# Turning x in the DMA, as two planes of 16-bit halves, in a pooled-attention and two-layer expert kernel

## The chip, the cores and the metric

The kernel runs on one core of one Trainium2 chip. A core has five engines that run side by side and wait for one another by semaphores: TensorE (matrix products, PE in the profile), VectorE (DVE), ScalarE (ACT), GpSimd (POOL) and SyncE (SP, which issues DMAs). The metric is the time of one execution in microseconds (us), as the median of several runs. Less is better.

## The reference, cut to what matters

```
s = scale * (q @ k.T);  a = softmax(s);  x = a @ v         # k = v = pooled kv @ w_sr, q is 24576 x 128

# expert layer 1, D = 128, E = 8 experts, F = 1024
logits = x @ w_gate;  e = argmax(logits);  gate = softmax(logits)[e]
x = gate * relu(x @ w1[e]) @ w2[e]

# expert layer 2: the same with its own weights, and one factor more
x = gate * sigmoid(x @ w_output_gate)[e] * relu(x @ w1[e]) @ w2[e]
```

Each token (a row of x, 128 numbers) goes to one expert, the one with the highest logit, and each layer is a pair of products with that expert's weights.

## The kernel before

**Stages.** Attention computes x in 96 blocks of 256 tokens. The two expert layers follow, each as up to 104 tiles of 256 tokens that all belong to one expert; 100 are in use here. Tokens get from the order of the input to the order of the experts through HBM: each row is scattered to a place in its expert's part of a bucket (x_bucket for layer 1, y_bucket for layer 2), and a tile is 256 consecutive rows of a bucket, read back. A row in a bucket is 768 bytes: 128 numbers of x, the token's number (ID) and its gate (GATE), and unused space. The last layer scatters its rows straight to the output.

**Precision by halves.** TensorE multiplies in a rounded 32-bit format. So each operand is kept as a rounded part and a rest (x_hi and x_lo, h_hi and h_lo, the weights likewise), and each product is made of three. ScalarE makes the rounded part (x_high, line 1503; h_high, line 1509), VectorE the rest (x_low, line 1712; h_low, line 1718).

**One tile, on TensorE** (tile_body). The products need x with the 128 features on the partitions, while a bucket's rows come with tokens on the partitions. So turn_x (lines 1279 to 1287) turns the tile's two blocks of 128x128 by two transposes into PSUM bank 5, from which x_high and x_low read. The up products of a tile come in four parts of six matmuls (up, line 1303), the down products in four of six (down, line 1320), then the result, copied by ScalarE to oT (yT_out, line 1517), is turned back into rows (tile_rows, lines 1335 and 1337: in layer 1 by a product that also gives the next layer's logits, in layer 2 by a transpose). The order in one body c is written out by hand: up 0 of tile c; down 2 and 3 of tile c-1; up 1 and 2; the rows of tile c-1; the turn of x for tile c+1; up 3; down 0 and 1. PSUM banks are taken by hand too.

**ScalarE, in order, in body c:** h_high 0; yT_out of tile c-1; h_high 1; x_high of tile c+1; h_high 2 and 3. **VectorE:** h_low 0 and 1; x_low of tile c+1; h_low 2 and 3; then the rows of tile c-1 times their gates (tile_rows_out, lines 1736 and 1738); between them the small steps of routing for the tokens of two blocks at a time (route), whose last step, place, is what a scatter waits for. **GpSimd:** the scatters (line 413 into the buckets, line 997 to the output), each as an indirect DMA of 128 rows, and during attention also the split of the weights into part and rest (lines 940 and 942), which SyncE stores in a table in HBM. **SyncE:** load_x (line 752) loads tile c+3 of x into one of four slots once the rows of tile c-1 are out; next_w loads weights of 1 MB where the expert changes.

Of the kernel before, what the change touches and what calls it, by code (L numbers as in the profile page):

```python
# [25 lines left out]
F32 = mybir.dt.float32  # L26
F32R = mybir.dt.float32r
BF16 = mybir.dt.bfloat16
I32 = mybir.dt.int32
ALU = mybir.AluOpType  # L30
# [10 lines left out]
PITCH = 132  # L41
LINE = 192
ID, GATE = 128, 129
LG = 16
# [28 lines left out]
def moe_kernel(nc, q, kv, w_sr, wg1, w1a, w2a, wg2, wog2, w1b, w2b, out):  # L73
# [36 lines left out]
    x_bucket = nc.dram_tensor("x_bucket", [E * STRIDE + BLOCK, LINE], F32, kind="Internal").ap()  # L110
    y_bucket = nc.dram_tensor("y_bucket", [E * STRIDE + BLOCK, LINE], F32, kind="Internal").ap()
# [4 lines left out]
    with ctx:  # L116
# [39 lines left out]
        rows = sb("rows", [P, 2, GSUB, LG + LINE])  # L156
# [15 lines left out]
        neutral = sb("neutral", [P, SUB, PITCH])  # L172
# [12 lines left out]
        rows_mid = kv_store[:, 0:2 * GSUB * (LG + LINE)].rearrange("p (g s c) -> p g s c", g=2, s=GSUB)  # L185
# [41 lines left out]
        sb("pad_xr", [P, 40])  # L227
        xr_slots = sb("xr", [P, 4, 384])
        xr = xr_slots[:, :, 0:SUB * PITCH].rearrange("p k (s c) -> p k s c", c=PITCH)

# [27 lines left out]
        class Route:  # L258


            def __init__(self, n):
# [3 lines left out]
                self.rows = rows if n == 1 else rows_mid  # L265
                self.place = places[n - 1]
# [17 lines left out]
                self.place_done = sem(f"place_done{n}")  # L284
                self.scattered = [[sem(f"scattered{n}_{g}_{h}") for h in range(2)] for g in range(2)]
# [16 lines left out]
        def route(dve, r, i, gc, name):  # L302
# [5 lines left out]
            logits = r.rows[:, g, :, LG - r.n * E:LG - r.n * E + E]  # L308
# [8 lines left out]
            if name == "skip":  # L317
                wait(dve, r.row_step, i, UNROLL * r.row_steps, r.row_steps * (2 * gc + 2))
                done(nc.vector.tensor_scalar(cand[:, :, E], r.rows[:, g, :, LG + ID].bitcast(I32), float(N), float(BIG),
# [30 lines left out]
            elif name == "opened":  # L350
                after("onehot")
                done(nc.vector.tensor_tensor(opened[:, :, :], r.rows[:, g, :, LG - E:LG], r.onehot[:, g], ALU.mult))
# [17 lines left out]
            elif name == "gate":  # L370
                after("den")
                nc.vector.reciprocal(r.rows[:, g, :, LG + GATE], den_g[:, 2])
# [26 lines left out]

        def scatter(pool, r, i, gc, h):  # L400

            if live(i, gc, r.groups, 2):
                g = gc % 2
                if h == 0:
                    wait(pool, r.place_done, i, 2, gc + 1)
                elif r.n == 1 and live(i, 2 * gc + 5, NBLK, UNROLL):

                    wait(pool, p_turned, i, PAIRS * UNROLL, PAIRS * (2 * gc + 5) + 2)
                else:
                    wait(pool, up_done, i - NIT if r.n == 1 else i, HP * UNROLL, HP * (2 * gc + 5) + 2)  # L410
                pool.sem_inc(r.scatter_go, 1)
                for s in range(h * SUB, (h + 1) * SUB):
                    nc.gpsimd.indirect_dma_start(  # L413
                        r.bucket[:, :], bass.IndirectOffsetOnAxis(r.place[:, g, s:s + 1], 0), r.rows[:, g, s, LG:], None,
# [219 lines left out]
        x_turned = sem("x_turned")  # L634
# [31 lines left out]
        with nc.Block(no_gpsimd_drain=True) as block:  # L666

            @block.sync
            def _(sp):
# [77 lines left out]
                def load_x(i, c, layer):  # L747
# [4 lines left out]
                    return sp.dma_start(xr[:, c % 4],  # L752
                                        layer.r.bucket[bass.ds(row, BLOCK), 0:PITCH].rearrange("(p s) c -> p s c", s=SUB))

                def next_x(i, c, n):

                    if live(i, c, limit[0], UNROLL):
                        wait(sp, row_step, i, RS * UNROLL, RS * (c - 3))
                        load_x(i, c, layer_of(i, c, n)).then_inc(x_in[c % 4], 16)
# [63 lines left out]
                load_x(0, 0, layers[1]).then_inc(x_in[0], 16)  # L823
                first_w(layers[1], 0, 0)
                load_x(0, 1, layers[1]).then_inc(x_in[1], 16)
                sp.wait_ge(p_turned, PAIRS * (NBLK - 2))
                first_w(layers[1], 0, 1)
                load_x(0, 2, layers[1]).then_inc(x_in[2], 16)
# [13 lines left out]
                with sp.Else():  # L842
                    limit[0] = TILES - UNROLL
                    for c in range(UNROLL):
# [3 lines left out]
                        if c:  # L848
                            wait(sp, row_step, TIT - 2, RS * UNROLL, RS * c)
                            load_x(TIT, c - 1, layers[2]).then_inc(x_in[c - 1], 16)  # L850
                        next_w(TIT - 2, c + 2, 1, sel, 1)
                    limit[0] = 2 * TILES
                    for k in range(UNROLL):
                        sp.wait_ge(x_in[k], 16 * (TIT - 1 + (k < 3)))
                        sp.sem_inc(x_in[k], 16)
# [13 lines left out]
            def _(pool):  # L869
# [20 lines left out]
                pool.memset(neutral[:, :, :], 0.0)  # L890
                pool.memset(rows[:, :, :, :], 0.0)
# [11 lines left out]
                for g in range(2):  # L903
                    pool.iota(rows[:, g, :, LG + ID].bitcast(I32), pattern=[[1, GSUB]], base=(g - 2) * GTOK,
# [928 lines left out]
```

## Time and profile before

| | |
|---|---|
| time, median of 3 runs | 1875.81 us (1872.98 to 1877.0) |
| the profiled execution, from its first to its last instruction | 2009.7 us |
| mean granted clock of TensorE, profiled | 0.986 |
| DMA | 185.88 MB, 92 GB/s on average |

The profiled execution is one other execution, and a longer one: its span is 133.9 us above the median of the runs, which is 0.933 of it. All durations of rows belong to that execution. In rows, "L1303" is line 1303 of the kernel, "out<-in" are tile names, "x1600" is a count; idle time is that of the engine just before the instruction, with what ended it. Matmuls overlap, so that their durations don't add up. "SPq" is an instruction of SyncE's queue. "remote" means that the profile names no instruction that ended the wait. "PEclk" is the granted share of TensorE's full clock.

### The profile page before, as it was taken

The page shows a single profiled execution, that of the slowest core. Times are in us where ns is not written, and L with a number is a line of the kernel's source. Part 1 is how long each engine was busy: PE and PEld are TensorE (multiplying, and loading weights), DVE is VectorE, ACT ScalarE, POOL GpSimd, SP SyncE. Part 2 cuts the span into 40 slices and gives each one's busy share as a digit, 9 for nine tenths or more (in the row PEclk, how much of TensorE's full clock was granted, in tenths as well). Part 3 has the DMA queues.
Part 4 walks back from the last instruction along what each step waited for, and adds up shares of the span by engine and source line. Part 5 has one row for each costly group of instructions (what it writes and reads, how often), then busy time and mean ns, then how long its engine had stood idle before and what let it go on. Part 6 is the DMA issues. An engine that isn't in the chain of part 4 may idle for free. (4 is left out here: it accounts for less than half of the span.)

```text
span 2009.7 us, 53289 instructions
## 1 busy us (share of the span) xinstructions
PE 1918.1 (95%) x15716; PEld 1879.5 (94%) x15716; DVE 1342.6 (67%) x3525; ACT 1054.8 (52%) x2333; POOL 739.4 (37%) x823
## 2 busy tenths in 40 slices
PE   9999999999999999998999989899999999999998
PEld 7999999999999989898898889888999999999998
DVE  6788887888887666565566666666655555555555
ACT  3777777777776344344344444343444444444444
POOL 5456643466643323222222222222333333333333
PEclk8999999999999999999999999999999999999999
DMA  8355532355533211111321111142211114141111
GB/s 301 104 169 174 178 102 74 109 172 175 173 114 125 67 49 50 42 46 44 118 92 44 45 48 42 51 135 74 66 44 46 43 42 165 42 163 43 46 44 36
DMA packets 138040, 185.88 MB, mean 92 GB/s; under 512 B 17425, under 2 KB 95380, under 8 KB 134368
## 3 DMA queue, kind: packets, MB, share of 16 engines
q1 hardware_dynamic: 112640, 134.16, 20.9%
q0 software_dynamic: 25312, 50.65, 7.1%
q8 instruction: 43, 0.70, 0.1%
q14 instruction: 45, 0.37, 0.1%
HBM read 98.41 MB, written 87.63 MB: 93 GB/s over the span
## 5 line engine op out<-in xcount | busy, mean ns | idle before, releaser
L1718 DVE SCALAR_TENSOR_TENSOR h_lo<-psum,h_hi 128x512 fp32r<-128x512 f32 x800 | 541.2, 688 | 248.3 <-ACT h_hi L1509 198.4
L1509 ACT ACTIVATE h_hi<-psum 128x512 fp32r<-128x512 f32 x800 | 460.6, 598 | 259.1 <-PE psum L1303 244.9
L1303 PE MATMUL psum<-x_hi,w 128*128 128x256 f32 x1600 | 344.7, 290 | 66.6 <-DVE x_lo L1712 48.7
L413 POOL DMA_INDIRECT y_bucket<-kv_store,place x200 | 194.3, 971 | 542.1 <-DVE place L379 484.5
L1303 PE MATMUL psum<-x_hi,w_split 128*128 128x256 f32 x1600 | 339.6, 287 | 9.2 <-issue 2.8
L997 POOL DMA_INDIRECT out<-rows x200 | 193.9, 970 | 405.0 <-DVE rows L1738 368.5
L1303 PEld LDWEIGHTS psum<-x_hi,w 128*128 128x128 f32 x1600 | 270.2, 192 | 75.5 <-issue 55.2
L1320 PE MATMUL psum<-h_hi,w 128*128 128x256 f32 x1600 | 321.6, 285 | 0.7 <-DVE h_lo L1718 0.7
L413 POOL DMA_INDIRECT x_bucket<-rows,place x192 | 190.0, 990 | 293.2 <-DVE place L379 197.7
L1303 PEld LDWEIGHTS psum<-x_hi,w_split 128*128 128x128 f32 x1600 | 265.5, 189 | 17.4 <-issue 10.5
L1320 PEld LDWEIGHTS psum<-h_hi,w 128*128 128x128 f32 x1600 | 266.4, 195 | 1.3 <-DVE h_lo L1718 1.3
L1712 DVE TENSOR_TENSOR x_lo<-psum,x_hi 128x256 fp32r<-128x256 f32 x200 | 84.8, 424 | 251.4 <-ACT x_hi L1503 194.9
L1608 DVE TENSOR_TENSOR pT_lo<-psum,pT_hi 128x512 fp32r<-128x512 f32 x288 | 197.5, 686 | 82.6 <-ACT pT_hi L1454 45.5
L1503 ACT ACTIVATE x_hi<-psum 128x256 fp32r<-128x256 f32 x200 | 76.7, 384 | 313.8 <-PE psum L1287 161.7
L1454 ACT ACTIVATE pT_hi<-psum 128x512 fp32r<-128x512 f32 x288 | 172.4, 599 | 107.0 <-PE psum L1175 100.8
L1320 PE MATMUL psum<-h_lo,w 128*128 128x256 f32 x800 | 227.4, 284 | 0.0
L1303 PE MATMUL psum<-x_lo,w 128*128 128x256 f32 x800 | 225.1, 281 | 0.0
L1303 PE MATMUL psum<-x_lo,w_split 128*128 128x256 f32 x800 | 222.8, 278 | 0.0
L1602 DVE TENSOR_REDUCE neg_max<-psum 128x1 f32<-128x768 f32 x192 | 182.0, 948 | 15.7 <-PE psum L1150 15.7
L1191 PE MATMUL psum<-pT_hi,kv_hi 128*128 128x256 f32 x576 | 185.9, 323 | 1.0 <-DVE pT_lo L1608 0.8
L1175 PE MATMUL psum<-ident,probs 128*128 128x128 f32 x1152 | 174.4, 274 | 1.2 <-DVE kv_lo L1585 1.1
L1445 ACT ACTIVATE probs<-psum,neg_max 128x768 f32<-128x768 f32 x192 | 172.3, 897 | 3.6 <-DVE neg_max L1602 3.6
(177 smaller groups left out, 4385.1 us busy)
## 6 DMA issues: line engine op xcount, KB each, us to landing
w_table<-w_split SPq DMA_DIRECT2D x64, 512.0 KB, 3.5
w_raw<-in_moe_w SPq DMA_DIRECT2D x64, 256.0 KB, 4.1
xr<-x_bucket SPq DMA_DIRECT2D x100, 132.0 KB
xr<-y_bucket SPq DMA_DIRECT2D x100, 132.0 KB
kv_store<-in_kv SPq DMA_DIRECT2D x24, 512.0 KB, 9.3
q_in<-in_q SPq DMA_DIRECT2D x48, 256.0 KB, 2.7
w<-w_table SPq DMA_DIRECT2D x12, 1024.0 KB, 6.8
w_split<-w_table SPq DMA_DIRECT2D x8, 1024.0 KB
```

The source lines that it names most:

```text
L413: nc.gpsimd.indirect_dma_start(r.bucket[:, :], bass.IndirectOffsetOnAxis(r.place[:, g, s:s + 1], 0), r.rows[:, g, s, LG:], None, bounds_ch ...
L997: nc.gpsimd.indirect_dma_start(out[:, :], bass.IndirectOffsetOnAxis(rows[:, g, s, LG + ID:LG + ID + 1].bitcast(I32), 0), rows[:, g, s, LG: ...
L1175: ins = nc.tensor.transpose(ps[:, m * BLOCK + s * P:m * BLOCK + (s + 1) * P], probs[:, c % 2, s, (2 * j + m) * P:(2 * j + m + 1) * P], ide ...
L1191: ins = nc.tensor.matmul(o_bank[:, 0:BLOCK], a[:, key, 1, :], b[:, j, at], start=j == m == n == 0, stop=j == PAIRS - 1 and m == 1 and n == 2)
L1303: ins = nc.tensor.matmul(bank[p][:, m * BLOCK:(m + 1) * BLOCK], layer.w1[c % 2][:, hl, f], x[:, c % 2, :], start=k == 0, stop=k == 2)
L1320: ins = nc.tensor.matmul(bank[4][:, 0:BLOCK], layer.w2[c % 2][:, hl, 2 * p + m, :], h[:, p, t], start=p == m == k == 0, stop=p == HP - 1 a ...
L1445: nc.scalar.activation(probs[:, c % 2, s, :].rearrange("p (m k) -> p m k", m=2), scores_ps(s), ACT.Exp, bias=neg_max[:, c % 2, s:s + 1], a ...
L1454: nc.scalar.activation(pT_hi[:, j, :], bank[4 + j % 2][:, :], ACT.Copy) \
L1509: nc.scalar.activation(h_hi[:, p, :], bank[p][:, :], ACT.Relu).then_inc(h_hi_done, 1)
L1602: nc.vector.tensor_reduce(neg_max[:, c % 2, s:s + 1], scores_ps(s), AX.XY, ALU.max, negate=True).then_inc(maxed, 1)
L1608: nc.vector.tensor_tensor(pT_lo[:, j, :], bank[4 + j % 2][:, :], pT_hi[:, j, :].bitcast(F32), ALU.subtract).then_inc(p_lo_done, 1)
L1718: nc.vector.scalar_tensor_tensor(h_lo[:, p, :], bank[p][:, :], 0.0, h_hi[:, p, :].bitcast(F32), ALU.max, ALU.subtract).then_inc(h_lo_done, 1)
```

## The change

Before a row is scattered, GpSimd now parts each of its 128 numbers into the low and the high 16 bits and puts them as two planes of 128 halves side by side (halve). The loads of x become transposing DMAs of 16-bit elements, which bring both planes with the features on the partitions (x_halves); the two numbers that are not x, ID and GATE, come by a small DMA of their own (tags). ScalarE then joins the halves into 32-bit numbers in SBUF (join_x writes x_whole, in the place of w_raw, which is free by then), and x_high and x_low read that in place of PSUM. turn_x goes away. The rows that ScalarE and VectorE write (pre_rows, pre_mid) are separate from the ones that are scattered, so that GpSimd copies from one to the other; the last layer's rows are still written straight into the ones that go out. Tokens of a tile are now spread as (s p) and not as (p s).

```diff
+        def halve(pool, r, i, gc):
+            if live(i, gc, r.groups, 2):
+                g = gc % 2
+                for h in range(2):
+                    at = slice(h * SUB, (h + 1) * SUB)
+                    wait(pool, r.row_step, i, UNROLL * r.row_steps, r.row_steps * (2 * gc + h + 1))
+                    pool.sem_inc(r.halve_go, 1)
+                    pool.tensor_copy(r.rows[:, g, at, 0:D].bitcast(U16).rearrange("p s (k d) -> p s k d", k=2),
+                                     r.pre[:, g, at, r.n * E:r.n * E + D].bitcast(U16)
+                                     .rearrange("p s (d k) -> p s k d", k=2)).then_inc(r.halved, 1)
...
         def scatter(pool, r, i, gc, h):
...
+                wait(pool, r.halved, i, 4, 2 * gc + h + 1)
...
                 def load_x(...):
-                    return sp.dma_start(xr[:, c % 4],
-                                        layer.r.bucket[bass.ds(row, BLOCK), 0:PITCH].rearrange("(p s) c -> p s c", s=SUB))
+                    sp.dma_start_transpose(x_halves[:, c % 4],
+                                           layer.r.bucket[bass.ds(row, BLOCK), 0:D].bitcast(U16)).then_inc(x_in[k], 16)
+                    sp.dma_start(tags[:, c % 4], layer.r.bucket[bass.ds(row, BLOCK), D:PITCH]
+                                 .rearrange("(s p) c -> p s c", p=P)).then_inc(tags_in[k], 16)
...
     GpSimd, attention (group) and layer 1:
                     pool.tensor_tensor(rid, rid, id_step[:, :], ALU.add).then_inc(ids_done, 1)
+                    halve(pool, r1, i, gc)
                     wait(pool, ids_done, i, 2, gc + 1)
...
                     for gc in range(2):
+                        halve(pool, r2, i, gc)
                         for h in range(2):
                             scatter(pool, r2, i, gc, h)
...
     TensorE:
                         tile_rows(i, c - 1, n)
-                        turn_x(i, c + 1)
                         up(i, c, 3, n)
...
     ScalarE:
+                def join_x(i, c):
+                    if tile_live(i, c):
+                        if at(i, c, 0):
+                            act.wait_ge(split_done[1], 2 * NPART * E)
+                        wait(act, x_in[c % 4], i, 16, 16 * (c // 4 + 1))
+                        wait(act, x_lo_done, i, UNROLL, c - 1)
+                        nc.scalar.activation(x_whole[:, c % 2, :].bitcast(U16).rearrange("p (t k) -> p k t", k=2),
+                                             x_halves[:, c % 4], ACT.Copy).then_inc(x_joined, 1)
...
                 def x_high(i, c):
                     if tile_live(i, c):
-                        wait(act, x_turned, i, UNROLL, c + 1)
+                        wait(act, x_joined, i, UNROLL, c + 1)
                         wait(act, up_done, i, HP * UNROLL, HP * (c - 1))
-                        nc.scalar.activation(x_hi[:, c % 2, :], bank[5][:, 0:BLOCK], ACT.Copy).then_inc(x_hi_done, 1)
+                        nc.scalar.activation(x_hi[:, c % 2, :], x_whole[:, c % 2, :], ACT.Copy).then_inc(x_hi_done, 1)
...
                         h_high(i, c, 0)
+                        join_x(i, c + 1)
                         yT_out(i, c - 1)
...
     VectorE, x_low and tile_rows_out:
-                        nc.vector.tensor_tensor(x_lo[:, c % 2, :], bank[5][:, 0:BLOCK],
+                        nc.vector.tensor_tensor(x_lo[:, c % 2, :], x_whole[:, c % 2, :],
...
+                        wait(dve, tags_in[c % 4], i, 16, 16 * (c // 4 + 1))
```

## Rows read from the trace of the kernel before

**Rows 1.** The page, part 1: busy time, share of the span, instructions.
```profile
PE 1918.1 (95%) x15716; PEld 1879.5 (94%) x15716; DVE 1342.6 (67%) x3525; ACT 1054.8 (52%) x2333; POOL 739.4 (37%) x823
```
**Rows 2.** Windows: length; busy of PE, PEld, DVE, ACT, POOL; PEclk; DMA share; GB/s.
```profile
0.00:645.00 645.00, 638.06 (x4931) 620.90 (x4932) 523.63 (x1292) 450.11 (x1028) 341.88 (x412) 0.99 0.45 151
645.00:1395.00 750.00, 680.15 (x5672) 667.73 (x5670) 468.66 (x1512) 311.02 (x715) 199.71 (x208) 0.97 0.21 65
1395.00:2005.00 610.00, 599.94 (x5115) 590.91 (x5115) 350.32 (x722) 293.66 (x592) 195.90 (x202) 1.00 0.21 65
```
**Rows 3.** The chain of work, from 1500 to 1560 us, by line.
```profile
by line: PE psum L1303 46.9%; PE psum L1320 42.0%; PE psum L1287 5.7%; PE psum L1337 3.6%; DVE x_lo L1712 0.7%; ACT x_hi L1503 0.7%; issue 0.4%
```
**Rows 4.** Two groups by line and shape: busy us, mean ns; idle before.
```profile
L1608 DVE TENSOR_TENSOR pT_lo<-psum,pT_hi 128x512 fp32r<-128x512 f32 x288 | 197.5, 686 | 82.6 <-ACT pT_hi L1454 45.5 <-issue 32.1
...
L1287 PE MATMUL psum<-ident,xr 128*128 128x128 f32 x400 | 76.3, 273 | 0.0
```
**Rows 5.** Timeline of layer 2: start us, us, instruction, idle before.
```profile
1603.69 0.55 SPq L752 DMA_DIRECT2D xr<-y_bucket  x1
...
1604.08 0.38 ACT L1517 ACTIVATE oT<-psum 128x256 f32<-128x256 f32 x1 [0.89 <-PE psum L1320]
...
1605.23 0.38 PE L1337 MATMUL psum<-ident,oT 128*128 128x128 f32 x2
...
1605.44 0.38 PE L1287 MATMUL psum<-ident,xr 128*128 128x128 f32 x2
...
1607.11 1.08 ACT L1509 ACTIVATE h_hi<-psum 128x512 fp32r<-128x512 f32 x2
...
1608.88 0.60 ACT L1509 ACTIVATE h_hi<-psum 128x512 fp32r<-128x512 f32 x1 [0.69 <-PE psum L1303]
...
1622.48 0.55 SPq L752 DMA_DIRECT2D xr<-y_bucket  x1
...
1626.93 0.60 ACT L1509 ACTIVATE h_hi<-psum 128x512 fp32r<-128x512 f32 x1 [0.68 <-PE psum L1303]
```
**Rows 6.** Waits from 645 to 1395 us: us in total, times, longest.
```profile
ACT x_hi L1503 <- remote: 137.3, 43, 4.0
...
PE psum L1303 <- DVE x_lo L1712: 48.7, 34, 2.0
```
**Rows 7.** Timeline of one tile of layer 1.
```profile
903.24 0.28 PE L1303 MATMUL psum<-x_hi,w 128*128 128x256 f32 x1
...
907.23 0.38 ACT L1503 ACTIVATE x_hi<-psum 128x256 fp32r<-128x256 f32 x1 [3.76 <-remote]
907.51 1.08 ACT L1509 ACTIVATE h_hi<-psum 128x512 fp32r<-128x512 f32 x2
...
908.13 1.29 DVE L1718 SCALAR_TENSOR_TENSOR h_lo<-psum,h_hi 128x512 fp32r<-128x512 f32 x2
908.20 0.38 PE L1303 MATMUL psum<-x_hi,w 128*128 128x256 f32 x1 [1.92 <-DVE x_lo L1712]
...
909.00 0.28 PE L1320 MATMUL psum<-h_hi,w 128*128 128x256 f32 x1
```
**Rows 8.** GpSimd's groups by line, the whole span.
```profile
L413 POOL DMA_INDIRECT y_bucket<-kv_store,place x200 | 194.3, 971 | 542.1 <-DVE place L379 484.5 <-issue 56.1 <-PE psum L1303 1.5
...
L942 POOL TENSOR_TENSOR w_split<-w_raw,w_split 128x512 fp32r<-128x512 f32 x64 | 82.7, 1292 | 5.5
L940 POOL CAST w_split<-w_raw 128x512 fp32r<-128x512 f32 x64 | 40.6, 635 | 0.0
```
**Rows 9.** DMA issues: KB each, median us from issue to landing.
```profile
kv_store<-in_kv SPq DMA_DIRECT2D x24, 512.0 KB, 9.3
q_in<-in_q SPq DMA_DIRECT2D x48, 256.0 KB, 2.7
w<-w_table SPq DMA_DIRECT2D x12, 1024.0 KB, 6.8
...
y_bucket<-neutral SPq DMA_DIRECT2D x8, 132.0 KB, 2.2
```

More of the change, by code:

```diff
@@ L29 @@
 I32 = mybir.dt.int32
+U16 = mybir.dt.uint16
 ALU = mybir.AluOpType
@@ L307, in route @@
             ns = len(r.steps)
-            logits = r.rows[:, g, :, LG - r.n * E:LG - r.n * E + E]
+            logits = r.pre[:, g, :, 0:E]
             def after(step):
@@ L413, in scatter @@
                     nc.gpsimd.indirect_dma_start(
-                        r.bucket[:, :], bass.IndirectOffsetOnAxis(r.place[:, g, s:s + 1], 0), r.rows[:, g, s, LG:], None,
+                        r.bucket[:, :], bass.IndirectOffsetOnAxis(r.place[:, g, s:s + 1], 0), r.rows[:, g, s, :], None,
                         bounds_check=E * STRIDE - 1, oob_is_err=False).then_inc(r.scattered[g][h], 16)
@@ L633, in moe_kernel @@
         x_in = [sem(f"x_in{k}") for k in range(4)]
-        x_turned = sem("x_turned")
+        tags_in = [sem(f"tags_in{k}") for k in range(4)]
+        x_joined = sem("x_joined")
         x_hi_done = sem("x_hi_done")
@@ L975, in _ @@
                         for gc in range(2):
+                            halve(pool, r2, i, gc)
                             for h in range(2):
@@ L981, in _ @@
                 with pool.Else():
+                    pool.wait_ge(r2.halved, 4 * (TIT - 2))
+                    pool.sem_inc(r2.halved, 4)
                     for gc in range(2):
+                        halve(pool, r2, TIT - 1, gc)
                         for h in range(2):
@@ L1278, in body @@
                             pe.wait_ge(kv_lo_done, NCHUNK)
-                def turn_x(i, c):
-                    if tile_live(i, c):
-                        if at(i, c, 0):
-                            pe.wait_ge(p_lo_done, PAIRS * (NBLK - 1) + 2)
-                        wait(pe, x_in[c % 4], i, 16, 16 * (c // 4 + 1))
-                        wait(pe, x_lo_done, i, UNROLL, c)
-                        for s in range(SUB):
-                            ins = nc.tensor.transpose(bank[5][:, s * P:(s + 1) * P], xr[:, c % 4, s, 0:D], ident[:, :])
-                        ins.then_inc(x_turned, 1)
                 def up(i, c, p, n):
@@ L1493, in body @@
                         if at(i, c, NBLK - 1):
+                            join_x(0, 0)
                             x_high(0, 0)
@@ L1727, in tile_rows_out @@
                         if layer.n == 1:
-                            to, skip = r2.rows, 0
+                            to, into, skip = r2.rows, r2.pre[:, g, h:h + SUB], 0
                             if not at(i, c, TILES - 1):
@@ L1731, in tile_rows_out @@
                         else:
-                            to, skip = rows, 2 * E
+                            to, into, skip = rows, rows[:, g, h:h + SUB, 0:D].bitcast(F32), 2 * E
                             if isinstance(i, int) and UNROLL * i + c < TILES + 4:
```

80 lines of the change are left out of this document (42 added, 38 removed).

## The prediction

> **What bounds the kernel now.** The page's first part comes first: TensorE is busy 95% of the span, twice ScalarE's share and far above GpSimd's [rows 1]. A share over the whole span hides stages, so the next view is the busy time by window [rows 2]. It shows three stages: attention (to 645 us), the first expert layer (645 to 1395) and the second (1395 to 2005). In the second TensorE is idle for 610 - 599.9 = 10 us only; in the first for 750 - 680.2 = 70 us, and the granted clock's mean is 0.97 there against 1.00. Then the chain of work that ended last, taken inside the second layer: it is TensorE alone but for about 2%, and the turns of x are 5.7% of it (they hold the chain whenever it goes through x_hi) [rows 3]. So in layer 2 an instruction taken off TensorE comes back as time; layer 1 needs a look at who ends its waits.
>
> **What is removed.** Two transposes per tile, 400 in all, 273 ns each [rows 4]. They overlap their neighbours, so 273 ns isn't their price. In layer 2, 5115 matmuls fill 599.9 us, 0.117 us each; a tile has 24 + 24 + 2 + 2 = 52 of them, so the stretch holds 98 tiles of 6.2 us. In layer 1 it is 680.2 / 5672 = 0.120 us [rows 2]. 400 x 0.118 = 47 us. The timeline gives 1605.44 - 1605.23 = 0.21 us for a pair of transposes [rows 5], 42 us for 200 tiles. I take -45 us, half in each layer.
>
> **What the removal does to waits.** x_hi (line 1503) no longer waits for TensorE, so x_lo and the next tile's up product don't either. In layer 1 TensorE stood 48.7 us in 34 waits for x_lo, behind x_hi, whose own wait has no named releaser for 137 us [rows 6]. One such case: x_hi starts only at 907.23, after 3.76 us of idle time, and TensorE resumes at 908.20 after 1.92 us [rows 7]. It is tempting to give all of that back. But the half h_hi that follows x_hi at 907.51 waits for the same late signals of TensorE: its product ended by 903.52 (903.24 + 0.28), yet ScalarE, idle for 3.76 us, had already passed that point in its order only for x_hi's sake. If the signal of the up product is as late as that of the turn, h_hi takes x_hi's place at 907.23, h_lo follows 0.62 us later (as 908.13 follows 907.51) and lasts about 0.69 us like pT_lo of its shape [rows 4], so the down product that needs it starts near 908.6 and not at 909.00. That is 0.4 us, 0.2 of which is the turns already counted. 34 cases x 0.2 = 7 us; in layer 2 I add 1. So -8 us; the ends are 0 and the whole 80 us of idle time. The next thing to be late is h_lo.
>
> **What is added on ScalarE.** join_x copies 128x512 halves, 200 times. The nearest row is h_hi, also 128x512, 0.60 us [rows 5]; gross 120 us. It stands between the first h_hi and the copy to oT. There ScalarE waits 0.89 us for TensorE (1604.08, [rows 5]), and back-to-back activations start about 0.5 us apart (two take 1.08 us). So it costs nothing while x has landed. Without that cover it is 200 x 0.5 = 100 us. ScalarE's load goes from 293.7 to about 350 of 610 us, far from bound. x_hi now reads SBUF instead of PSUM: no such row, taken as equal.
>
> **What is added on GpSimd.** halve, one per tile or block: 96 for layer 1's rows, 100 for layer 2's, each 128x512 halves. Rows nearby: a cast 128x512 635 ns, a two-input one 1292 ns [rows 8]; I take 1 us, 200 us gross. GpSimd is 53% busy in the first 645 us and 27% in layer 1 [rows 2], and before scatters it idles for the places that VectorE computes, 484.5 us in all before those into y_bucket [rows 8]. A block's rows are ready before its place is, so halve falls into that idle time: 0 us. Queued behind it are only scatters (and weight splits in attention), which have blocks to spare.
>
> **What changes in the DMAs.** SP issues two DMAs per tile for one: the transposing load and the tags. One issue is 0.55 us [rows 5]; SP issues about once a tile of 6.2 us, so a second one, and a longer first, fit. More matters how long the load takes. Before, x is needed at the turn late in a body; now ScalarE needs it right after the first h_hi. The timeline has one load issued at 1603.69 whose join point is the end of h_hi at 1608.88 + 0.60: 5.8 us. The shorter case is 1622.48 to 1626.93 + 0.60: 5.05 us [rows 5]. About a period less 0.6 us in layer 2, and over a microsecond more in layer 1. How long a transposing load takes no row shows. Nearest rows: 132 KB of the same row form land in 2.2 us, 256 KB in 2.7 us, 1 MB in 6.8 us, 512 KB beside other loads in 9.3 us [rows 9]. The payload is 128 KB in 512 pieces of 256 B, so I take the low side, 4 us, with ends 2.2 and 9.3. At 4 us it is hidden. If it lands late, the join is late by w = L - (T - 0.6), where T is the period; the copy to oT then has about 0.3 us left before it and its consumer starts 0.77 us after it ends (1604.46 to 1605.23), so about 1.1 us of w costs nothing. Where a 1 MB weight load (6.8 us) goes ahead of x, the join may stall; for the few tiles at a change of expert I add +4 us (ends 0 and 20).
>
> **Sum.** -45 - 8 + 4 = -49 us on the profiled span of 2009.7 us. The unprofiled median is 1875.8 us, so the same work goes 0.933 as long; -49 x 0.933 = -46, and 1875.8 - 46 = 1830 us. By the end values of the hidden costs alone, this case lies between 1800 and 1855.
>
> **Rivals.**
> - *The turned load lands late.* Against it: the short landings of similar size [rows 9]. For it: the load is cut into small pieces, and no row shows one. With T0 = 6.2 - 0.23 = 5.97 us the late join gives T = T0 + w - 1.1, so T = (T0 + L - 0.5) / 2. L = 8.5 us gives 6.99 us in layer 2, +79 us over 100 tiles; in layer 1 (7.5 - 0.27 = 7.23 us) it gives 7.6, +11 us. Together +90 us, 1960 us unprofiled. At L = 6.8 it is still faster (6.14 us in layer 2, 1848 us); the sign turns near 7.5 us, and L = 9.3 gives about 2034 us. Chance 0.18.
> - The Trainium skill has a rule that speaks for this rival: "VectorE: DVE Perf Modes", section "The three transpose paths", gives 390 ns for a 128x128 turn of 2-byte data on TensorE and 1309 ns through the DMA crossbar, and its rules for kernel authors send such a turn to TensorE when the result may lie in PSUM. Four such blocks are 5.2 us, an estimate from that page; on top of the landing of an ordinary load that is 7.4 us, and the time would come out near no change. No row of before can test it.
> - *The waits of layer 1 go as a whole.* If TensorE's signal of the up product isn't late, only that of the turn, the 70 us of idle time shrinks by some 45: 1830 - 42 = 1788 us. For it: x_hi alone shows the unnamed releaser in quantity [rows 6]. Against it: h_hi is issued behind x_hi and so can't show its own. Chance 0.10.
> - *An engine beside TensorE gets slower.* GpSimd's 200 copies run beside VectorE, whose h_lo is the next to be late; if each copy held up one 0.69 us instruction, half of them on the path, it is +69 us, 1895 us. Against it: in attention, where the casts of before ran, VectorE's pT_lo takes 686 ns [rows 4], and an h_lo without them 0.69 us of the same shape (the span of two is 1.29 us, [rows 7]). Chance 0.05.
> - *The gain is eaten*: joins and late loads at changes cost what the turns give. Within 0.2%. Chance 0.05.
>
> **Numbers.** My forecast has 0.62. Faster than by 0.2% (about 4 us, what a measurement can tell from no change): 0.62 + 0.10 = 0.72; same 0.05; slower 0.18 + 0.05 = 0.23. The range 1795 to 1920 leaves out the strongest form of the second rival and most of the first one's; the likeliest case's own is 1800 to 1855.
>
> **What the new profile would show.** Right: no group of line 1287's form; TensorE's chain in layer 2 as before without it, period near 5.97 us; the join starting right after h_hi and oT's wait shorter by about 0.5 us; x_lo no longer a releaser of TensorE, h_lo one in layer 1. Wrong: the join waiting on the DMA tile after tile, or the transposing load shown landing later than 6 us; h_hi, h_lo or the copies on GpSimd longer than 0.60, 0.69 and 1.3 us; more stretches at half clock.

## The result, and the profile after

The changed kernel takes 1843.9 us (1843.0 to 1845.4, four runs) where the kernel before takes 1876.4 (1873.0 to 1877.6, four runs): a ratio of 0.9835, with an interval from 0.9823 to 0.9847, 32 us less. The forecast was 46 us less. The profiled execution of the changed kernel has a span of 1841.9 us. Part 1 of its page, against [rows 1]:

```profile
PE 1817.3 (99%) x15316; PEld 1797.2 (98%) x15316; DVE 1358.6 (74%) x3525; ACT 1195.9 (65%) x2533; POOL 856.0 (46%) x1019
```

TensorE is busy 99% of the span and has 400 instructions fewer; ScalarE and GpSimd have 200 and 196 more. The 70 us of idle time in layer 1 that [rows 2] show is absent. Its windows (attention, layer 1, layer 2), with the columns of [rows 2]:

```profile
0.00:645.00 645.00, 636.65 (x4983) 620.69 (x4984) 534.25 (x1303) 459.87 (x1039) 394.70 (x508) 1.00 0.45 153
645.00:1250.00 605.00, 601.00 (x5307) 598.39 (x5307) 477.80 (x1476) 371.43 (x792) 254.09 (x299) 1.00 0.29 77
1250.00:1842.00 592.00, 579.63 (x5030) 578.13 (x5028) 346.60 (x749) 364.65 (x702) 207.18 (x213) 1.00 0.26 67
```

The groups of what was added (ScalarE's over the window 1250 to 1842, GpSimd's over the span), beside which h_hi, once 0.60 us [rows 5], has stayed:

```profile
L1534 ACT ACTIVATE h_hi<-psum 128x512 fp32r<-128x512 f32 x400 | 238.4, 596 | 205.6 <-PE psum L1321 201.9 <-PE psum L1338 1.4
L1521 ACT ACTIVATE w_raw<-x_halves 128x512 uint16<-128x512 uint16 x99 | 77.5, 783 | 0.1
...
L415 POOL COPY kv_store<-kv_store 128x512 uint16<-128x512 uint16 x100 | 59.2, 632 | 4.0 <-DVEq L1829 2.2 <-DMA x_bucket<-rows,place 1.9
L415 POOL COPY rows<-pre_rows 128x512 uint16<-128x512 uint16 x96 | 56.0, 613 | 3.5 <-ACT pre_rows L1484 3.5
```

The join (L1521) lasts 0.78 us and has almost no idle time before it: in layer 2 x has landed each time. The same place as [rows 5] in the timeline of layer 2, ScalarE's and SyncE's rows:

```profile
1386.31 0.60 ACT L1534 ACTIVATE h_hi<-psum 128x512 fp32r<-128x512 f32 x1 [1.44 <-PE psum L1321]
1386.80 0.78 ACT L1521 ACTIVATE w_raw<-x_halves 128x512 uint16<-128x512 uint16 x1
1387.67 0.38 ACT L1542 ACTIVATE oT<-psum 128x256 f32<-128x256 f32 x1
...
1386.78 1.23 SPq L773 DMA_TRANSPOSE x_halves<-y_bucket  x1
1388.20 0.42 SPq L775 DMA_DIRECT2D tags<-y_bucket  x1
```

The copy to oT (1387.67) follows the join directly, where before it had waited 0.89 us [rows 5]. The load issued at 1386.78 is joined at 1392.57, 5.8 us later. In the trace its 512 packets of 256 bytes end at 1388.88, and the last of its 16 signals, for which the join waits, comes at 1389.66, 2.9 us after the issue began. Over the whole trace the median of this landing is 3.0 us (168 of the 200 loads, those whose signals can be told apart). The plain load of the kernel before, read in the same way from an ordinary execution (first experiment), lands after 2.6 us.

### The profile page after: what moved, and what is told of

It reads as the page before. It is cut to its first block and busy times, and to the rows that moved or that the text cites. A ratio compares the mean times of both kernels' runs of the same rounds, so it can differ in the third digit from the quotient of the medians.

```text
span 1841.9 us, 53814 instructions
## 1 busy us (share of the span) xinstructions
PE 1817.3 (99%) x15316; PEld 1797.2 (98%) x15316; DVE 1358.6 (74%) x3525; ACT 1195.9 (65%) x2533; POOL 856.0 (46%) x1019
## 5 line engine op out<-in xcount | busy, mean ns | idle before, releaser
L1746 DVE SCALAR_TENSOR_TENSOR h_lo<-psum,h_hi 128x512 fp32r<-128x512 f32 x800 | 548.9, 689 | 321.5 <-ACT h_hi L1534 316.1
L1534 ACT ACTIVATE h_hi<-psum 128x512 fp32r<-128x512 f32 x800 | 476.4, 596 | 426.8 <-PE psum L1321 423.1
L1321 PE MATMUL psum<-x_hi,w_split 128*128 128x256 f32 x1600 | 332.8, 284 | 5.1 <-DMA w_split<-w_table 3.3
L1321 PE MATMUL psum<-x_hi,w 128*128 128x256 f32 x1600 | 332.3, 283 | 3.5 <-DMA w<-w_table 3.2
L1338 PE MATMUL psum<-h_hi,w 128*128 128x256 f32 x1600 | 305.0, 276 | 0.0
L1321 PEld LDWEIGHTS psum<-x_hi,w 128*128 128x128 f32 x1600 | 264.0, 188 | 4.1 <-issue 2.2
L1338 PEld LDWEIGHTS psum<-h_hi,w 128*128 128x128 f32 x1600 | 255.9, 188 | 0.0
L1338 PE MATMUL psum<-h_lo,w 128*128 128x256 f32 x800 | 221.0, 276 | 0.0
L1221 PE MATMUL psum<-pT_hi,kv_lo 128*128 128x256 f32 x576 | 160.8, 279 | 0.0
L1221 PE MATMUL psum<-pT_lo,kv_hi 128*128 128x256 f32 x576 | 160.7, 279 | 0.0
```

The lines of the kernel that those rows point to most:

```text
L1221: ins = nc.tensor.matmul(o_bank[:, 0:BLOCK], a[:, key, 1, :], b[:, j, at], start=j == m == n == 0, stop=j == PAIRS - 1 and m == 1 and n == 2)
L1321: ins = nc.tensor.matmul(bank[p][:, m * BLOCK:(m + 1) * BLOCK], layer.w1[c % 2][:, hl, f], x[:, c % 2, :], start=k == 0, stop=k == 2)
L1338: ins = nc.tensor.matmul(bank[4][:, 0:BLOCK], layer.w2[c % 2][:, hl, 2 * p + m, :], h[:, p, t], start=p == m == k == 0, stop=p == HP - 1 a ...
L1534: nc.scalar.activation(h_hi[:, p, :], bank[p][:, :], ACT.Relu).then_inc(h_hi_done, 1)
L1746: nc.vector.scalar_tensor_tensor(h_lo[:, p, :], bank[p][:, :], 0.0, h_hi[:, p, :].bitcast(F32), ALU.max, ALU.subtract).then_inc(h_lo_done, 1)
```

## The experiments

**A measure by layer.** SyncE issues one load of x per tile, so the first and the last start of a layer's 100 loads give that layer's time (99 tiles). The trace lists them by instruction: duration least/median/most in ns, then the two starts. First the kernel before (an ordinary execution, first experiment), then the changed one:

```profile
L752 SPq DMA_DIRECT2D xr<-x_bucket x100: 549/554/693, 615.0 to 1251.9; - x100
L752 SPq DMA_DIRECT2D xr<-y_bucket x100: 543/554/655, 1259.0 to 1847.0; - x100
```
```profile
L773 SPq DMA_TRANSPOSE x_halves<-x_bucket x100: 1203/1222/1397, 615.0 to 1232.8; - x100
L773 SPq DMA_TRANSPOSE x_halves<-y_bucket x100: 1210/1222/1378, 1240.7 to 1816.7; - x100
```

Layer 1 takes 636.9 and then 617.8 us (-19.1), layer 2 takes 588.0 and then 576.0 (-12.0). All kernels, read in the same way:

| kernel | time before there | its time | ratio (interval) | layer 1 | layer 2 |
|---|---|---|---|---|---|
| before | 1875.5 | 1874.3 | 0.9996 (0.9986 to 1.0007) | 636.9 | 588.0 |
| changed | 1876.4 | 1843.9 | 0.9835 (0.9823 to 0.9847) | 617.8 | 576.0 |
| turns kept | 1875.5 | 1887.9 | 1.0060 (1.0046 to 1.0073) | 646.7 | 589.8 |
| join twice | 1875.5 | 1845.0 | 0.9835 (0.982 to 0.985) | 618.7 | 575.3 |
| weights first | 1875.5 | 1854.3 | 0.9880 (0.9862 to 0.9899) | 622.3 | 583.2 |
| one turn | 1877.3 | 1865.3 | 0.9939 (0.9925 to 0.9953) | 633.4 | 581.2 |
| *second kind of chip:* before (first profile) | | | | 736.5 | 617.9 |
| changed | 1995.2 | 1921.9 | 0.9634 (0.9618 to 0.9649) | 679.3 | 588.6 |
| turns kept | 1995.2 | 1933.4 | 0.9700 (0.9681 to 0.9719) | 676.0 | 602.4 |
| one turn | 1991.6 | 1908.8 | 0.9579 (0.9557 to 0.9602) | 663.4 | 591.6 |
| tags last | 1991.6 | 1914.2 | 0.9613 (0.9589 to 0.9636) | 673.0 | 586.4 |
| loads twice | 1995.2 | 1930.2 | 0.9670 (0.9643 to 0.9697) | 681.1 | 598.9 |
| x_hi late | 1991.6 | 1931.7 | 0.9698 (0.9675 to 0.9722) | 681.4 | 596.4 |
| halve twice | 1991.6 | 1934.4 | 0.9710 (0.9681 to 0.9739) | 686.7 | 588.7 |

The kernel before takes 1875 to 1877 us on some chips of this type and 1991 to 1995 us on two others. Kernels are compared within a kind only, by their ratios to the kernel before on the same chip. Of the second kind, changed, turns kept and loads twice ran on the chip with 1995.2 us; one turn, tags last, x_hi late and halve twice ran on the one with 1991.6, where the changed kernel did not. So a difference between these two groups also holds what differs between the two chips. The layers' times are of one execution each. On which chip the first profile of before was taken isn't known; its span of 2009.7 us is like the second kind's.

**1. Before, once more.** No edit.

> The kernel before, unchanged, for a second profile. The execution profiled first was 2009.7 us long, against 1876 us in the runs, with 78 us of idle TensorE time in layer 1 behind x_lo. Theory A: that was one odd execution, and an ordinary one has a span near 1874 us, layer 1 at about 6.2 us a tile with under 10 us of idle TensorE time, so that there were no waits behind x_hi for the change to give back. Theory B: the stalls belong to every execution of this kernel and only the profiler's load lengthens them; the profile is again near 2010 us. The time of this run is 1876 us within 0.2% under both.

Measured: a span of 1872.1 us, and 602.97 us busy of the 605 from 645 to 1250 us. TensorE's waits in that window (us, times, longest):

```profile
PE psum L1303 <- DMA w<-w_table: 2.0, 2, 1.4
```

The 48.7 us of waits for x_lo [rows 6] aren't there. The waits on which the prediction put 8 us belong to the execution of the first profile and not to those whose median it forecast.

**2. Turns kept.** Two transposes per tile ahead of the row products; the output is the same.

```diff
+                        for s in range(SUB):
+                            nc.tensor.transpose(bank[5][:, s * P:(s + 1) * P], oT[:, c % 2, s * P:(s + 1) * P], ident[:, :])
```

> The changed kernel with two transposes per tile put back on TensorE: they turn oT into PSUM bank 5, from which nothing reads, ahead of the row products. Everything else of the change stays (DMA transpose, halve, join). Theory A: a pair costs 0.21 us, 200 tiles give +42 us, about 1886 us, so 10 us above the kernel before: the rest of the change then costs 10 us. Theory B: a pair costs only 0.16 us and nothing else changed the time, +32 us, 1876 us. Theory C: TensorE has slack now and they are hidden, under +10 us.

Measured: 44 us above the changed kernel (42 by the ratios), 12 us above before. So on this kind of chip nothing is gained while TensorE has as many instructions as before: the gain comes with the turns that are gone. The 12 us are not all a price of the rest of the change, for with the turns kept most tiles of layer 1 run at a slower pace of TensorE (below).

**3. One turn**, the same edit with a single transpose, run on a chip of each kind.

> The changed kernel with one transpose of oT per tile (200 in all, into an unused part of a bank) ahead of the row products; the output is unchanged. With two of them (the experiment that keeps the turns) the time was 1887.9 us, 44 us above the changed kernel's 1843.9. Theory: the price of a transpose is its place in TensorE's stream, 0.11 us each, so one gives half, +22 us, 1866 us. Rival: a part of the 44 us is a price of the first one (the switch between kinds of matmul) or of the waits around it; then one gives 30 us or more, 1874 us or above. Other side: the first is free and the second costs it all, 1850 us or less.

> The changed kernel with one transpose of oT per tile added, run again. Where the kernel before takes about 1991 us, it gave a ratio of 0.9579, below the changed kernel's own 0.9634 there. If that is a property of such chips (the transpose fills idle time in layer 1, and TensorE's stream after the row products runs at 113 ns a matmul instead of 118 in every third tile of layer 2), then a chip of that kind gives 0.955 to 0.961 again. On a chip where before takes about 1875 us, nothing is idle in layer 1 and the transpose costs: +11 to +22 us against the changed kernel's 1844, that is 1855 to 1866 us (ratio 0.989 to 0.995). Rival: the one transpose helps there as well, 1844 us or less, and a version of the changed kernel with one transpose would be the better kernel.

Measured: on the first kind +21 us, half of what two cost, as a price by the place in TensorE's stream would have it. By layer it is less clean: one turn costs 15.6 us in layer 1 and 5.2 in layer 2, two cost 28.9 and 13.8, where 0.11 us a turn would give 11 and 22 in each; the rest is TensorE's changing pace (below). On the second kind the kernel with one turn has a ratio 0.0055 below that of the one with none, which would be 11 us *faster*, but on the other chip. In the profiled executions layer 1 is 16 us shorter (663.4 against 679.3) and layer 2 3 us longer. The expected 1866 us was wrong there, for layer 1 isn't bound by TensorE's stream on that kind.

**4. Join twice.** ScalarE does each join a second time, into an unused buffer.

```diff
+                        nc.scalar.activation(x_other[:, c % 2, :].bitcast(U16).rearrange("p (t k) -> p k t", k=2),
+                                             x_halves[:, c % 4], ACT.Copy)
```

> The changed kernel with each join done twice on ScalarE (the first into a spare place), 0.78 us more per tile ahead of the copy to oT. Theory A: the join of 0.78 us just fills the wait that oT had, and the reserve behind it is about 0.7 us, so the second one costs little: 0 to +40 us (up to 0.2 us a tile). Rival: the reserve is already used up by the first join, and the second shows in full, 200 x 0.7 = +140 us, which would mean that the first join costs time too.

Measured: 1845.0 us, the same ratio to four digits. 155 us more of work on ScalarE cost nothing; the join is hidden with 0.8 us to spare.

**5. Weights first.** SyncE issues both weight loads of 1 MB ahead of x and its tags.

```diff
-                        next_x(i, c + 3, n)
                         next_w(i, c + 2, n, sel, 1)
+                        next_x(i, c + 3, n)
```

> The changed kernel with SyncE's order altered: in each body the second weight load is issued ahead of the load of x and not behind it. The profile of the changed kernel has TensorE waiting 7.5 us for weights at six places, and periods near them above the usual 5.75 and 6.04 us. Theory A: the transposing load (1.22 us to issue, 0.42 us more for the tags) makes the weight loads behind it late, and this order gives back 3 to 8 us, about 1838 us. Rival: the second weight load waits for the down product, so x is issued later than before and its landing of 2.9 us no longer fits into the lead of 5 us; slower by 10 us or more.

Measured: 10 us slower than the changed kernel. (The changed kernel's waits for weights, 7.5 us in what was expected, are 6.5 us at six places in the view: 3.2 in layer 1 and 3.3 in layer 2.) Its timeline at a change of expert, SyncE's queue and then ScalarE:

```profile
1532.78 0.35 SPq L808 DMA_DIRECT2D kv_hi<-w_table  x1
1534.21 1.29 SPq L773 DMA_TRANSPOSE x_halves<-y_bucket  x1
...
1541.27 0.77 ACT L1521 ACTIVATE w_raw<-x_halves 128x512 uint16<-128x512 uint16 x1 [3.54 <-DMA x_halves<-y_bucket]
```

Issued at 1534.21 behind weight loads, x is there at 1541.2 only, 7 us later, and the join waits 3.5 us. That is the prediction's first rival, made to happen at some places: 15 joins wait, 24 us together, and TensorE waits nine times for the copy to oT behind them, 8.3 us. But it isn't the landing by itself that is new. Beside the weight loads the changed kernel's x lands as late (7.2 us after its issue at 1225.32), and so does the plain load of before (7.0 us at one place). What this order takes away is the lead: from the issue to the point at which ScalarE is ready for the join the median is 5.8 us in the changed kernel and 4.2 here, since x is issued only behind the second weight load and what that waits for. In the changed kernel one join waits 1.9 us, at 704 us, where SyncE had stored neutral rows ahead of that load. A part of the 10 us is TensorE's clock: its granted mean is 0.996 here against 0.999.

**6. The changed kernel again**, on a chip of the second kind, together with **turns kept**.

> The changed kernel, unchanged, run beside the two others here. The last four kernels ran on another chip of the same kind, on which the kernel before takes 1991.6 us and not 1875.5, and TensorE waits in layer 1 for signals that come late, as in the first profile of before. Expected by the theory that the prediction's waits of layer 1 are a property of the chip: where the kernel before takes about 1991 us, the changed kernel takes 1905 to 1920 us (ratio 0.957 to 0.964), 70 us or more gained; where it takes about 1875 us, 1844 us (0.983). Rival: the four kernels of the last batch were all slowed or sped by their own edits, and the changed kernel keeps its ratio of 0.983 everywhere, 1958 us where before takes 1991.

> The changed kernel with two transposes of oT per tile added on TensorE ahead of the row products (200 pairs, output unchanged), as in the second experiment. On a chip where before takes about 1875 us: 1888 us (ratio 1.006), as measured. On one where it takes about 1991 us: by the theory that layer 1's period is set there by late signals and the turns only fill idle time, the turns cost their 22 us in layer 2 and little in layer 1, so 1910 to 1935 us; by the rival that they stand in the path in both layers, 44 us above the changed kernel there.

Measured: ratio 0.9634, 73 us gained, and just 11.5 us lost with the turns kept: 13.8 in layer 2, nothing in layer 1 (676.0 against 679.3). In layer 1 of this kind the turns only fill idle time. So 62 of the 73 us are gained with the turns still on TensorE: on this kind most of the gain isn't TensorE's instructions. That x_hi no longer waits for TensorE would explain it, and the rows below fit; no run separates this from the rest of the change. One tile of its layer 1, rows of GpSimd, TensorE and ScalarE:

```profile
904.39 0.99 POOL L433 DMA_INDIRECT y_bucket<-kv_store,place  x1 [6.95 <-DVE place L386]
...
908.39 0.99 POOL L433 DMA_INDIRECT y_bucket<-kv_store,place  x1 [0.30 <-issue]
```
```profile
906.46 0.28 PE L1321 MATMUL psum<-x_hi,w 128*128 128x256 f32 x1
...
911.50 0.38 PE L1338 MATMUL psum<-h_hi,w 128*128 128x256 f32 x1 [1.54 <-DVE h_lo L1746]
```
```profile
910.13 1.08 ACT L1534 ACTIVATE h_hi<-psum 128x512 fp32r<-128x512 f32 x2 [3.13 <-PE psum L1321]
```

The first of the two h_hi (part 2) needs the up product that ended at 906.46 + 0.28 = 906.74. ScalarE is free from 907.0, but h_hi starts at 910.13, 3.1 us late, while GpSimd issues its four scatters. TensorE then stands for h_lo. This is the tile of [rows 7] with h_hi in x_hi's place, as the prediction drew it. In the whole of layer 1 (645 to 1310 us) TensorE's waits are:

```profile
PE psum L1338 <- DVE h_lo L1746: 45.4, 41, 1.6
PE psum L1321 <- DMA w<-w_table: 2.0, 2, 1.3
```

**7. Tags last.** SyncE issues the tags behind the second weight load.

```diff
-                        next_x(i, c + 3, n)
+                        row = next_x(i, c + 3, n)
                         next_w(i, c + 2, n, sel, 1)
+                        if row is not None:
+                            load_tags(row, c + 3, layer_of(i, c + 3, n), (c + 3) % 4)
...
```

> The changed kernel with SP issuing a tile's tags behind the second weight load, instead of between the transposing load and that load. TensorE waits for weights 3.6 us in layer 1 and 3.9 us in layer 2 in the changed kernel, 2.3 and about 0 in the kernel before. Theory: SP's longer issues (1.22 us for the transposing load and 0.42 us for the tags against 0.55 us for one load) make the second weight load late, so 0.42 us less per change of expert gives back 1 to 3 us, 1841 to 1843 us. Rival: the wait is for the weights' transfer itself beside the transposing load, and the time stays at 1844 us. Third: the tags are late for the row's copy on VectorE, and the time goes above 1846 us.

Measured: 0.9613 against 0.9634, with intervals that overlap and on two chips. Perhaps 4 us better; not settled, and not measured on the first kind, for which the three times were forecast.

**8. Loads twice.** A second transposing load per tile into an unused buffer, issued first.

```diff
+                    wait(sp, spare_in[k], i - back, 16, 16 * (c // 4))
+                    sp.dma_start_transpose(x_spare[:, c % 4],
+                                           layer.r.bucket[bass.ds(row, BLOCK), 0:D].bitcast(U16)).then_inc(spare_in[k], 16)
...
```

> The changed kernel with a second transposing load of the same rows per tile, into an unused buffer and ahead of the real one in SP's queue. The real one then lands about 1.2 us later or more than the 2.9 us after its issue that the trace of the changed kernel shows, so about 4.1 to 5 us after the point at which it was issued before, against a lead of about 5 us. Theory: the load and its double still lie inside the lead, the join waits little, and only weights at a change of expert come later: 0 to +15 us against the changed kernel on the same chip. Rival (the late load of the prediction): the crossbar takes the two one after the other, the join waits tile after tile and the time rises by 30 us or more.

Measured: 8 us more than the changed kernel on the same chip. In the profiled executions, which are 12 us apart, layer 1 takes 1.8 us more and layer 2 10.3. ScalarE's group has 22 us of waits, at eleven of the joins (up to 3.3 us) and not one per tile:

```profile
L1526 ACT ACTIVATE w_raw<-x_halves 128x512 uint16<-128x512 uint16 x194 | 151.6, 782 | 22.2 <-DMA x_halves<-x_bucket 11.2 <-DMA x_halves<-y_bucket 8.2 <-SPq L884 2.6
```

Layer 2 of the changed kernel and of this one, with the columns of [rows 2]:

```profile
1306.30:1894.90 588.60, 575.16 (x4950) 572.41 (x4950) 349.07 (x749) 364.74 (x696) 200.76 (x206) 0.99 0.26 68
1309.30:1908.20 598.90, 581.65 (x4955) 578.83 (x4954) 346.64 (x747) 362.58 (x695) 202.00 (x207) 0.98 0.37 88
```

6.5 of the 10.3 us are TensorE's own busy time, for as many matmuls, at a lower granted clock (0.98 against 0.99); 3.8 are idle time. The transposing path has room for a load more per tile; mostly the lead isn't used up.

**9. x_hi late.** x_high behind h_high 2, x_low behind h_low 2.

```diff
-                        x_high(i, c + 1)
                         h_high(i, c, 2)
+                        x_high(i, c + 1)
...
```

> The changed kernel with x_hi moved behind the third h_hi on ScalarE and x_lo behind the third h_lo on VectorE. In the changed kernel's second layer a down product is issued every 114.7 ns against 113.3 ns in the kernel before, though nothing there waits; 50 of them per tile make 0.07 us per tile, about 6.5 us over the layer. Theory P: this comes of which reads and writes of the other engines fall beside which products, so another order of x_hi and x_lo moves it: the layer's pitch falls to 113.3 ns and the time to about 1838 us (or it goes up as much). Theory Q: it comes of the transposing load's own traffic, and the pitch stays at 114.4 to 115.2 ns and the time at 1844 us. If x_lo is late for the next tile's up product, TensorE shows waits for x_lo and the time is above 1850 us.

Measured: ratio 0.9698 against 0.9634, 13 us slower, on the other chip. TensorE waits for x_lo (26 us in layer 1), as the last sentence of what was expected has it. The pitch in layer 2 did not fall (115.1 ns in the mean of the tiles against 114.8). That is theory Q's range, but Q's cause isn't borne out: one turn (experiment 3) has the same transposing load and 113.5 ns there. Nor is P refuted, for which tiles are slow did change. The experiment doesn't decide between them.

**10. Halve twice**, for the rows that go into y_bucket, the second time into an unused buffer.

```diff
+                    if r.n == 2:
+                        wait(pool, r.halved, i, 4, 2 * gc + h)
+                        pool.sem_inc(r.halve_go, 1)
+                        pool.tensor_copy(spare[:, :, :].rearrange("p s (k d) -> p s k d", k=2), ...
```

> The changed kernel with GpSimd's parting copy done twice for every block that goes into y_bucket (100 blocks, about 0.62 us each; the additional copy goes into an unused buffer). Prediction's theory: the copies lie in GpSimd's idle time ahead of the scatters and cost nothing, so 1844 us, ratio about 0.983, and h_lo on VectorE stays at 0.69 us. Rival: GpSimd's copies hold up VectorE or make scatters late; if one copy costs half of a VectorE instruction of 0.69 us on the path, 100 more of them give +35 us, 1879 us, and more than 3 us above 1844 would already show that halve is not free.

Measured: ratio 0.9710 against 0.9634, which would be +15 us, but on another chip of the second kind. 7.4 us of it lie in layer 1, where the copies are, 4.7 ahead of its first load (623.0 against 618.3 us), where nothing was added. h_lo lasts 690 ns as in the others. So VectorE's instruction isn't held up. But TensorE's waits for h_lo in layer 1 are 53.7 us against 45.4, about as much more as the layer takes, and whether the additional copies or the chip cause this isn't known. Whether halve costs some microseconds on this kind stays open, and on the first kind it wasn't tried. There only the changed kernel's own trace speaks for a hidden halve: its first load of x starts at 615.0 us as before, with 88 of the 96 copies for layer 1's rows ahead of it, and in neither layer does TensorE wait for GpSimd.

## Why the prediction was right or wrong

**The mechanism held** on the kind of chip whose time was forecast. TensorE is the bound, the two turns were on its path, and they came back as time. The turned load is early, the join is hidden (experiment 4), and halve as far as the trace shows. The sum was 14 us too large. By its steps:

**Turns removed, -45: the price of a pair is right, its return in layer 2 is not.** In the chain of work of the kernel before, in an ordinary execution, the pair (L1287) holds 0.22 us; 200 of them make 44. In layer 1 the mean period of the undisturbed tiles fell from 6.27 to 6.04 us, by just that. In layer 2 it fell from 5.91 to 5.76, by 0.15 only. (The prediction's factor of 0.933 made 42 of its 45; the price of a pair is the same in the short execution, so the factor had nothing to scale there.) The chain of the changed kernel in layer 2 shows the rest (start, us, pieces):

```profile
1458.26 0.71 PE psum L1321 x6
1458.96 1.36 PE psum L1338 x12
1460.32 0.68 PE psum L1321 x6
1461.00 1.36 PE psum L1338 x12
1462.36 1.36 PE psum L1321 x12
1463.73 0.22 PE psum L1355 x2
1463.94 0.71 PE psum L1321 x6
1464.65 1.41 PE psum L1338 x12
1466.07 0.71 PE psum L1321 x6
1466.77 1.41 PE psum L1338 x12
1468.19 1.42 PE psum L1321 x12
1469.60 0.22 PE psum L1355 x2
1469.82 0.71 PE psum L1321 x6
```

After the row products (L1355) TensorE issues its next six matmuls at 118 ns each (0.71 us). Mostly it then goes over to 113 ns (1.36 us for twelve). In every third tile it doesn't: 1463.94 to 1469.82 is 5.88 us where the tile ahead of it takes 5.68, and TensorE waits for nothing. That is 0.07 us per tile on average, 7 us in layer 2. Counted over the layer, 31 of 100 tiles are such; the kernel before has 2 of 100 there, and so has the one with one turn:

```profile
1452.51 0.22 PE psum L1337 x2
1452.72 0.22 PE psum L1287 x2
1452.94 0.70 PE psum L1303 x6
1453.64 1.36 PE psum L1320 x12
```

(kernel before, again in layer 2). With the turns kept it is layer 1 in which most tiles run at 118 ns (73 of 100; 49 with one turn, 2 in the changed kernel), so that layer 1 lost 28.9 us by two turns and layer 2 13.8. That the sum is near 44 us, in the second experiment and in half for one turn, is luck in part: the pace costs in one layer what it gives back in the other. What decides between the two paces isn't settled: another order on ScalarE and VectorE changed which tiles are slow but not the mean (experiment 9), and the transposing load alone isn't it, for the kernel with one turn has that too.

**Waits given back, -8: nothing, on the chips whose time was forecast.** The prediction read 34 waits from a profile 134 us longer than the median and scaled its sum by 0.933. An ordinary execution has none of them. On the second kind they are real, and there the step was too small: layer 1 fell by 57.2 us, though the turns are worth nothing in it. Layer 1 of the kernel before (first profile), with the turns kept and of the changed kernel, and one stretch of the first:

```profile
622.60:1359.10 736.50, 670.35 (x5588) 657.50 (x5587) 464.47 (x1496) 312.93 (x718) 197.00 (x207) 0.98 0.22 69
618.20:1294.20 676.00, 655.92 (x5576) 644.58 (x5575) 467.63 (x1495) 380.24 (x816) 259.61 (x309) 1.00 0.27 73
618.30:1297.60 679.30, 628.68 (x5383) 615.26 (x5383) 465.20 (x1495) 378.63 (x816) 259.57 (x309) 1.00 0.27 73
817.70:821.10 3.40, 3.40 (x18) 3.40 (x17) 2.01 (x8) 1.06 (x3) 0.00 (x0) 0.50 0.06 13
```

TensorE's idle time is 66 us before, 20 with the turns kept and 51 without them. So with equal work on TensorE 46 us of idle time went (if the first profile is of this kind of chip), which is the size that the prediction's rival named (the waits of layer 1 go as a whole, 45 us); in the changed kernel h_hi's late starts show as waits again, since the turns no longer fill them. That h_hi inherits x_hi's waits is what the rows of experiment 6 show. So both were half right: h_hi inherits them, but each is shorter than the chain of turn, x_hi and x_lo was.

A second part of the 57 us had no term in the prediction, which had read the clock's mean of 0.97 in layer 1. In that layer TensorE's granted clock is at 0.50, the lower of its two levels, in ten stretches, as in the last row, where it does 18 matmuls in 3.4 us; the two waits for x_lo in the 28 us ahead of that row are 3.1 us. With the turns kept and in the changed kernel the layer's mean is 1.00. An estimate from the layer's mean of 0.98 is 15 us of its 736.5. The runs agree: on the chip with 1995.2 us the median of the mean clocks is 0.990 for before and 0.997 for changed, by which 14 of the 73 us would be the clock.

**Late loads at a change of expert, +4: right in size, wrong in place.** Behind the weight loads x does land late, up to 7.2 us after its issue. But the tiles are longer there too: wherever x lands after more than 5.5 us, ScalarE comes to the join 6.7 us or more after the issue, and none of these joins waits more than 0.1 us. (The one wait of 1.9 us is elsewhere.) Instead TensorE itself waits for late weights: 3.2 us in two waits in layer 1 (2.0 before), and in layer 2, where there were none:

```profile
PE psum L1321 <- DMA w_split<-w_table: 3.3, 4, 1.2
```

With the idle time around them that makes about 5 us (TensorE's idle time rises from 2.6 to 5.8 us in layer 1 and from 2.1 to 5.1 in layer 2, the later start below included). SyncE's transposing issue of 1.22 us and the tags' 0.42 stand ahead of the second weight load where 0.55 us stood [rows 5]; experiment 7 fits that but doesn't show it. One term was left out: the first tile's x_hi starts at 639.4 us and not at 637.9, +1.5.

**The new sum:** -44 (pairs) + 7 (the slow pace) + 5 (weights) + 1.5 (start) = -30.5 us. The spans differ by 30 us (1872.1 to 1841.9), the medians by 32.

**Sizes taken from neighbours.** The join is 0.78 us and not 0.60; halve 0.61 to 0.63 where 1 was taken; the landing 3.0 us in the median where 4 was taken, below the 7.5 at which the sign was to turn. The estimate worked out from "VectorE: DVE Perf Modes", "The three transpose paths", in the Trainium skill (5.2 us for four blocks, 7.4 with an ordinary landing) isn't borne out: the whole landing of such a load is 2.9 us here. The measurement decides. And its advice to turn on TensorE names a price for the turn, not for TensorE being the bound.

## What to carry to other kernels

Before a trace's waits are priced, compare its span with the median that is to be forecast: waits in an execution 7% longer may belong to that chip alone, and scaling the sum doesn't remove them. Look at the clock's mean as well: what a stretch at the lower level costs stands in no list of waits. Where one engine is 99% busy, an instruction taken off it returns about its place in the stream (0.11 us here, but for the pace of the others) and not its duration (0.27). A transfer that takes over such work costs only where it lands behind its lead. So count the lead first, see what stands ahead of the transfer in its queue, and see what it stands ahead of.

## What the runs showed of the hardware

- **Two kinds of chip.** The same kernel takes 1875 or 1991 us. On the slower kind an h_hi of ScalarE can start 1.5 to 3.4 us after both its up product and ScalarE's instruction before it have ended. In layer 1 of the changed kernel's trace there are 42 such places with 104 us together, on the first kind there is none of over 1 us. At each of them GpSimd is issuing an indirect DMA; that this causes it was seen side by side, not tested, and GpSimd issues the same DMAs on the first kind. The change is worth 32 us on the one and 73 us on the other.
- **TensorE's pace.** At a granted clock of 1.00 and with no wait, the same matmul comes each 113 or each 118 ns, the slower pace for at least the first few after the row products, and for whole tiles in patterns that an added transpose moves (every third tile of layer 2 with none, every second of layer 1 with one, three of four there with two). The cause is open.
- **TensorE's clock.** On the slower kind it falls to 0.50 in short stretches, ten in layer 1 of the first profile, which has 66 us of idle time there, and in none in that layer of the changed kernel, which has 51 us. What brings it down wasn't tested.
- **A transposing DMA of 256x256 16-bit elements** (128 KB) takes SyncE 1.22 us to issue, against 0.55 for the plain load [rows 5], and lands 3.0 us after the issue began, against 2.6. Beside loads of 1 MB both take up to 7 us (7.2 and 7.0).
- **A ScalarE copy of 128x512 16-bit elements** that writes every other half takes 0.78 us, a 32-bit activation of as many elements 0.60.
